# Loading w_in two steps at a time, in chunks of 512 columns

## The reference, cut to what matters

```python
def _moe_ref(x, w_in, w_out):                 # x (1536, 512), w_in (512, 2048), w_out (2048, 512)
    h = x @ w_in
    g = np.where(h > 0.0, h, 1.0 * (np.exp(np.minimum(h, 0.0)) - 1.0))
    return (g @ w_out).astype(np.float32)

def _moe2_ref(x, expert_emb, tau, w1, w2):    # w1 (8, 512, 1024), w2 (8, 1024, 512)
    ...
    for e in range(E):
        mask = expert_idx == e
        h = np.maximum(x[mask] @ w1[e], 0.0)
        out[mask] = gate_w[mask, None] * (h @ w2[e])
```

## Time and profile before

| | us |
|---|---|
| median of 3 runs | 546.83 |
| lowest and highest | 546.75, 547.37 |
| the profiled execution's own time | 546.45 |
| its span, first to last instruction | 544.7 |
| PE busy | 532.5 |
| DVE busy | 301.7 |
| ACT busy | 234.0 |
| POOL busy | 82.0 |

### The profile page before, as it was taken

How to read it: one execution, slowest core, us unless ns; L and a number is a source line. 1 busy time by engine, 2 the same in 40 slices (tenths; PEclk the granted TensorE clock), 3 DMA queues, 4 the chain that set the end, 5 groups by cost and what they waited for, 6 DMA issues and landing times.

```text
span 544.7 us, 11801 instructions
## 1 busy us (share of the span) xinstructions
PE 532.5 (98%) x3930; PEld 458.7 (84%) x3931; DVE 301.7 (55%) x667; ACT 234.0 (43%) x530; POOL 82.0 (15%) x210
## 2 busy tenths in 40 slices
PE   8799999999999999999999999999999999999995
PEld 7688888888888888888889898888788888888883
DVE  3789887544644464447542557667583274322552
ACT  5677764443544453444332436461171251211440
POOL 6312020011100000000000000110312131111221
PEclk9999999999999999999999999999999999999999
DMA  9999322232121112110100720010875155101000
GB/s 208 275 273 315 91 48 64 54 75 71 50 64 24 25 25 64 25 25 15 40 1 2 266 84 0 20 59 2 309 256 185 44 206 188 39 28 35 19 19 24
DMA packets 63499, 49.23 MB, mean 90 GB/s; under 512 B 46038, under 2 KB 52182, under 8 KB 63456
## 3 DMA queue, kind: packets, MB, share of 16 engines
q1 hardware_dynamic: 61056, 42.36, 27.1%
q0 software_dynamic: 2400, 6.30, 3.5%
HBM read 43.40 MB, written 6.82 MB: 92 GB/s over the span
## 4 chain that ended last, share of the span: by engine, by line
PE 97%; ACT 1%; issue 1%; DVE 0%; POOLq 0%; DVEq 0%; ACTq 0%
PE bank L976 25%; PE bank L1020 8%; PE bank L1027 8%; PE bank L1033 8%; PE bank L1188 5%; PE bank L1234 5%; PE bank L1242 5%; PE bank L1196 5%; PE bank L1190 5%; PE bank L1236 5%; PE bank L954 3%; PE bank L936 2%; PE bank L927 2%; PE bank L1226 2%; PE bank L1086 1%; PE bank L832 1%
## 5 line engine op out<-in xcount | busy, mean ns | idle before, releaser
L1395 ACT ACTIVATE el<-bank 128x512 f32<-128x512 f32 x48 | 28.7, 597 | 106.0 <-PE bank L976 105.7
L1700 DVE TENSOR_SCALAR el<-el 128x512 f32<-128x512 f32 x48 | 20.7, 431 | 87.8 <-ACT el L1395 87.8
L976 PE MATMUL bank<-x_hi,w_hi_parts 128*128 128x256 f32 x376 | 60.9, 283 | 0.0
L976 PE MATMUL bank<-x_hi,w_lo_parts 128*128 128x256 f32 x376 | 60.4, 282 | 0.0
L976 PE MATMUL bank<-x_lo,w_hi_parts 128*128 128x256 f32 x376 | 60.2, 282 | 0.0
L976 PEld LDWEIGHTS bank<-x_hi,w_hi_parts 128*128 128x128 f32 x376 | 53.6, 188 | 3.2 <-issue 0.2
L1020 PE MATMUL bank<-w_hi_parts,g_hi 128*128 128x512 f32 x192 | 54.9, 408 | 0.0
L1027 PE MATMUL bank<-w_lo_parts,g_hi 128*128 128x512 f32 x192 | 52.8, 397 | 0.0
L1033 PE MATMUL bank<-w_hi_parts,g_lo 128*128 128x512 f32 x192 | 52.5, 395 | 0.0
L976 PEld LDWEIGHTS bank<-x_lo,w_hi_parts 128*128 128x128 f32 x376 | 51.5, 189 | 0.0
L976 PEld LDWEIGHTS bank<-x_hi,w_lo_parts 128*128 128x128 f32 x376 | 51.3, 188 | 0.0
(11 more groups left out here) (282 smaller groups left out, 917.6 us busy)
## 6 DMA issues: line engine op xcount, KB each, us to landing
raw<-in_moe_w SPq DMA_DIRECT2D x8, 2048.0 KB, 8.9
w_raw<-in_moe_w_in SPq DMA_DIRECT2D x8, 512.0 KB, 7.4
w_raw<-in_moe_w_out SPq DMA_DIRECT2D x8, 512.0 KB, 7.6
k_raw<-in_k SPq DMA_DIRECT2D x16, 192.0 KB, 3.2
v_raw<-in_v SPq DMA_DIRECT2D x8, 384.0 KB, 4.3
x_rows<-x SPq DMA_DIRECT2D x6, 512.0 KB, 4.1
q_raw<-in_q SPq DMA_DIRECT2D x44, 64.0 KB, 2.9
vwin<-in_v SPq DMA_DIRECT2D x32, 72.0 KB, 2.8
```

The lines of the kernel that those rows point to most:

```text
L976: mm = pe.matmul(o, r32(w[:, at:at + P]), r32(x[i % 2][:, c, :]), start=(part == "hh" and c == 0), stop=(part == "lh" and c == DC - 1))
L1395: act.activation(el[n % 2], bank[:, H_BANK[n % 2], :], ACT.Exp).then_inc(e_act, 1)
```

## The change

Steps 2j and 2j+1 of w_in share 2048 columns of SBUF: four chunks of 512 columns, in each the 256 columns of the one step and behind them the 256 of the other. Steps 2 and 3, 4 and 5, 6 and 7 are each loaded by one transfer of 1 MB, at the place at which the even one was loaded; the issues of the odd ones go. Steps 0 and 1 are still loaded alone, into the new places. ACT's split of an odd step waits for the pair's semaphore. Splits go over four pieces of 256 columns with a stride of 512 in place of 1024 in a row. PE reads the same tiles at new addresses. Pieces k of the first expert's weights now need both steps of a pair to be done in the last block: the wait is for the pair's second step, and piece 6 is split at the turn of piece 7 (n = 46, before n = 45).

```diff
--- before.py
+++ after.py
@@ -137,7 +137,7 @@
 
     def star_at(k):
 
-        return NS - 6 + k // 2 if k < CHUNKS - 1 else NS - 2
+        return NS - 6 + k // 2 if k < CHUNKS - 2 else NS - 2
 
     GATE_TILES = (slice(0, STAR_TILES), slice(STAR_TILES, NT))
 
@@ -460,8 +460,16 @@
         def vw_landed(u):
             return 16 * sum(vw_loads(x) for x in range(u % PAIRS, u + 1, PAIRS))
 
+
+        def w_in_at(s, c, a):
+
+            return s // 2 * 2 * CHUNK + (4 * c + s % 2 * 2 + a) * P
+
+        def w_in_pair(w, s):
+            return w[:, s // 2 * 2 * CHUNK:(s // 2 + 1) * 2 * CHUNK].rearrange("p (c f) -> p c f", c=DC)
+
         def w_in_part(w, s):
-            return w[:, s * CHUNK:(s + 1) * CHUNK]
+            return w_in_pair(w, s)[:, :, s % 2 * 2 * P:(s % 2 + 1) * 2 * P]
 
         def w_out_part(w, s):
             return w[:, WIN_SZ + s * 2 * DM:WIN_SZ + (s + 1) * 2 * DM]
@@ -511,8 +519,14 @@
                     sp.dma_start(vwin[lo - key0:hi - key0, g, w, :].rearrange("p (h d) -> p h d", h=2),
                                  vh[head:head + 2, lo:hi, :].rearrange("h p d -> p h d")).then_inc(ld_vw[g], 16)
 
+            def load_two_w_in(s):
+
+                sp.dma_start(w_in_pair(w_raw, s),
+                             w_in[:, s * 2 * P:(s + 2) * 2 * P].rearrange("(c p) f -> p c f", p=P)
+                             ).then_inc(ld_win[s], 16)
+
             def load_w_in(s):
-                sp.dma_start(w_in_part(w_raw, s).rearrange("p (c f) -> p c f", c=DC),
+                sp.dma_start(w_in_part(w_raw, s),
                              w_in[:, s * 2 * P:(s + 1) * 2 * P].rearrange("(c p) f -> p c f", p=P)
                              ).then_inc(ld_win[s], 16)
 
@@ -561,23 +575,20 @@
             load_w_in(1)
             load_w_out(0)
             load_q(5)
-            load_w_in(2)
+            load_two_w_in(2)
             load_windows(4)
             load_w_out(1)
-            load_w_in(3)
             load_windows(5)
             load_w_out(2)
             load_q(6)
-            load_w_in(4)
+            load_two_w_in(4)
             load_windows(6)
             load_w_out(3)
             load_q(7)
-            load_w_in(5)
             load_windows(7)
             load_w_out(4)
-            load_w_in(6)
+            load_two_w_in(6)
             load_w_out(5)
-            load_w_in(7)
             load_w_out(6)
             load_w_out(7)
             sp.wait_ge(m_mm, PAIRS)
@@ -972,7 +983,7 @@
                         if i == 0 and part == "lh":
                             pe.wait_ge(w_lo_v, low_made("in", s))
                         for c in range(DC):
-                            at = s * CHUNK + (2 * c + a) * P
+                            at = w_in_at(s, c, a)
                             mm = pe.matmul(o, r32(w[:, at:at + P]), r32(x[i % 2][:, c, :]),
                                            start=(part == "hh" and c == 0), stop=(part == "lh" and c == DC - 1))
                 mm.then_inc(h_mm, 1)
@@ -987,7 +998,7 @@
                     pe.wait_ge(vs_ev, 2)
                 pe.wait_ge(xl_ev, c + 1)
                 for a in range(2):
-                    w = r32(W_HI[:, (2 * c + a) * P:(2 * c + a + 1) * P])
+                    w = r32(W_HI[:, w_in_at(0, c, a):w_in_at(0, c, a) + P])
                     pe.matmul(rows_of_first(a), w, r32(x_hi[0][:, c, :]), start=(c == 0 and a == 0), stop=False)
                     pe.matmul(rows_of_first(a), w, r32(x_lo[0][:, c, :]), start=False, stop=False)
 
@@ -996,7 +1007,7 @@
                 pe.wait_ge(w_lo_v, low_made("in", 0))
                 for c in range(DC):
                     for a in range(2):
-                        mm = pe.matmul(rows_of_first(a), r32(W_LO[:, (2 * c + a) * P:(2 * c + a + 1) * P]), r32(x_hi[0][:, c, :]),
+                        mm = pe.matmul(rows_of_first(a), r32(W_LO[:, w_in_at(0, c, a):w_in_at(0, c, a) + P]), r32(x_hi[0][:, c, :]),
                                        start=False, stop=(c == DC - 1 and a == 1))
                 mm.then_inc(h_mm, 1)
 
@@ -1382,7 +1393,7 @@
 
             def split_high(kind, s):
                 if kind == "in":
-                    act.wait_ge(ld_win[s], 16)
+                    act.wait_ge(ld_win[s if s < 2 else s // 2 * 2], 16)
                     act.copy(r32(w_in_part(W_HI, s)), w_in_part(w_raw, s)).then_inc(w_hi_a, 1)
                 else:
                     act.wait_ge(ld_wout[s], 16)
@@ -1437,7 +1448,7 @@
 
             def star_high(k):
                 act.wait_ge(ld_w1 if k < CHUNKS // 2 else ld_w2, 16)
-                act.wait_ge(h_mm, STEPS * (NB - 1) + k + 1)
+                act.wait_ge(h_mm, STEPS * (NB - 1) + k // 2 * 2 + 2)
                 act.copy(r32(W_HI[:, k * CHUNK:(k + 1) * CHUNK]), raw[:, k * CHUNK:(k + 1) * CHUNK]
                          ).then_inc(star_hi, 1)
```

## The result

| | before | after |
|---|---|---|
| median, us | 547.12 (5 runs, 546.75 to 548.47) | 549.57 (5 runs, 548.97 to 550.53) |
| ratio of the runs, 95% interval | | 1.0037 (1.0025 to 1.005) |
| the profiled execution's own time | 546.45 | 549.2 |
| its span | 544.7 | 547.5 |

What follows compares the result with a forecast made beforehand. PE, 97% of the chain, was taken to bound the kernel. Profiled 546.45 us plus a 0.7 stall at project(2), other terms nothing, gave 547.15; carried to the median, 547.5, range 546.6 to 548.2.

Steps and rivals of the forecast that it cites:

- the price D of half a megabyte: Load queue ahead of w_out 3: the added half megabyte makes it 1.2 us later, 1.93 at the upper bound.
- D - 0.52: Low part of project(2): PE stalls for w_out 3's delay less a 0.52 us margin, 0.7 us.
- the place, the path and the margin: Late w_out 3 delays g_hi(2), g_lo(2), low split of w_out 2; PE stalls in project(2) beyond 0.52 us.
- a range that stopped at the mean rate: Upper end of the time: 272 GB/s, mean from 26 to 46 us, gives 1.93 us delay, 1.4 us stall.
- Undervalued: w_out 1: Before project(1): w_out 1 lands 1.3 to 1.9 us later, ACT waits 0.3 to 0.9, margin 0.64, cost nothing.
- Rival 2: Moved half megabyte costs the stretch's mean rate: w_out 3 1.93 us late, project(2) stall 1.4, 548.2 us; chance 0.18.
- Rival 1: Stall at project(2) hidden because w_out 3 comes less than 0.5 us late: 546.8 us; chance 0.22.
- rival 3: At the start, 1 KB packets were the brake and the start gets shorter: 545.7 us; chance 0.03.
- The rule of the Trainium skill: Load queue: about 2.0 us fixed per DMA, so one transfer fewer ahead of w_out 3 would prevent the stall.
- the splits in four pieces: w_in splits on ACT and DVE over four pieces: at most 0.03 us more for 1024 elements, cost nothing.
- expert piece 6: End of last block: its split moves one step back, covered by 0.5 us; nothing, or 0.1 to 0.3 us.
- SP's queue: SP's load issues: three fewer of about half a microsecond each, no PE wait on its later loads, cost nothing.

Runs made afterwards that it cites:

- changed again: The changed kernel run and profiled again, unedited, beside the kernel before: 548.69 us in 11 runs, ratio 1.0025.
- two adjacent singles: Changed kernel with each pair issued as two adjacent 512 KB loads at the pair's place: 549.93 us, ratio 1.0040 to the kernel before.
- first pair apart: Changed kernel with w_in 2 and 3 as single loads at their old places, other pairs joined: 549.13 us, ratio 1.0038 to the kernel before.
- windows behind moved: Changed kernel with windows 5 moved behind w_out 2 and windows 7 behind w_out 4: 550.29 us, ratio 1.0045 to the kernel before.
- windows ahead moved: Changed kernel with windows 4 moved directly behind w_out 1 and windows 6 behind w_out 3: 547.0 us, ratio 0.9989 to the kernel before.
- layout alone: Changed kernel with eight single w_in loads at their old places, new layout and piece 6 move kept: 547.99 us, ratio 1.0003 to the kernel before.

## Why the prediction was wrong

The mechanism was right and one term of its sum, the price D of half a megabyte, was too small by half. Loss against D, start offsets taken off (us). The step of the prediction said: loss = D - 0.52.

| kernel | D | D - 0.52 | loss measured |
|---|---|---|---|
| changed | 2.59 | 2.07 | 2.09 |
| changed again | 2.36 | 1.84 | 1.86 |
| two adjacent singles | 3.35 | 2.83 | 2.85 |
| first pair apart | 2.75 | 2.23 | 2.24 |
| windows behind moved | 1.94 | 1.42 | 1.44 |
| windows ahead moved | 1.38 | 0.86 | 0.88 |
| layout alone | 0.81 | 0.29 | 0.31 |

**Right: the place, the path and the margin.** PE stalls at the low part of project(2), released by the low split of w_out 2, through g_lo(2) and g_hi(2) from ACT's wait for w_out 3. The margin of 0.52 us held within 0.02 in seven profiles, and moving the split out of that path took the stall away.

**Wrong: the price of half a megabyte, D = 1.2 us.** It measured 2.6 and 2.4 us in two profiles (in the first with 0.6 that w_out 2 had too). I had taken the rate of a stretch in which w_in and w_out loads stood alone (366 and 381 GB/s), "since the moved bytes are w_in's". But here the rate wasn't a property of the bytes moved; it was one of the stretch into which they were moved: with the windows out of it, the same pair cost 1.5 us on its own landing and 2.1 on that of w_out 3, and no time. Even the mean of that stretch, 272 GB/s, taken as the upper bound, was too low a price at 1.93. The trace of before had a nearer row, the landing of w_in 3:

```profile
L515 SPq DMA_DIRECT2D w_raw<-in_moe_w_in x1: 471/471/471, 26.7 to 26.7; - x1
...
DMA to landing us min/median/max: 7.8/7.8/7.8
```

It landed at 26.7 + 7.8 = 34.5, 2.4 us behind w_out 1, which landed at 32.1. That spacing gives D = 2.4, a loss of 1.9 and 548.7 us for the median. The forecast gave single landings and didn't take their differences in that stretch.

**Wrong: a range that stopped at the mean rate.** That mean was no upper bound, since it averages over slices of 225 to 335 GB/s. One of the slow ones in the trace of the kernel before:

```profile
32.00:34.00 2.00, 2.00 (x17) 1.86 (x16) 1.67 (x4) 2.00 (x3) 0.00 (x0) 1.00 1.22 225
```

At 225 GB/s half a megabyte takes 2.3 us (an estimate), close to the 2.4 of the second profile. Windows close behind a load may add to its delay: in the new order they stand directly behind w_out 1, where w_in 3 stood before, and behind w_out 3 only query 7 is left between, where w_in 5 was too. The runs suggest that and don't show it.

**Undervalued: w_out 1.** The forecast saw the wait in front of it, with 0.64 us of margin in project(1), and priced it at nothing. With a landing 2.9 us late, it made project(1)'s low part 42.94 - 0.70 - 41.02 = 1.2 us late (0.7 in the second profile), and 1.3 to 1.5 where it alone was in the way. It adds nothing to the total only because w_out 3's delay is larger.

**Rival 2** (slower, D past 1.6) is what happened, on its mechanism, at a chance of 0.18; its 548.2 was below. **Rival 1** (the stall hidden) and **rival 3** (faster, with 1 KB packets as the brake) are out by the time and the stall. Something of rival 3's mechanism may be there: with adjacent 1 KB loads D was larger than with pairs, by 0.75 us and in one profile each. The rule of the Trainium skill that was weighed there (page "DMA: Bandwidth & Descriptors", section "Anatomy of one DMA — SWDGE (gpsimd) path"), which the page gives for loads issued by GpSimd while these are SP's, made w_out 3 earlier by joining; it came 2.4 to 2.6 us later, so at this place order outweighed whatever joining saves. **Nothing, as forecast:** the splits in four pieces, expert piece 6, SP's queue, w_in 2 and the pair 4 and 5 as such.

## What to carry to other kernels

Price a load that is moved in a queue by the spacing of landings in the stretch it is moved into, not by the best rate of its kind elsewhere, and look which small-piece loads stand ahead of it. An in-order engine turns a wait into a delay of all that stands behind the waiting instruction: when a wait is late, see first whether the work behind it can go ahead of it, which here took a few lines and gave all of the loss back. The two late deliveries to the same engine didn't add up here; only the larger delay at the last meeting place counted.

## What the runs showed of the hardware

- The queue's rate fell by more than half, from 377 or more to 143 to 174 GB/s, while the value windows (pieces of 256 bytes for 96 partitions) were moved, with its engines busy all the time; a query load's pieces of 256 bytes for 128 partitions, mixed with large ones, left it at 328 (by the estimate above 1 ns for a small piece against 1.7). Whether the 96 partitions, the source's order or something else makes the difference wasn't tried.
- A load of 0.19 MB of such pieces moved from ahead of a 512 KB load to behind it brought the landing forward by 1.9 to 2.4 us, four times its bytes at 381 GB/s.
- Executions with identical instructions ahead of it begin project(0) up to 1.3 us apart (start offsets from -0.06 to 1.22). In the one with 1.22 the loads of w_in 1 and w_out 0 had landed 2 us late; what causes the others wasn't found.
